# q and k of the first four units by one transfer each, the maximum of k from two turned rows, embeddings later, new order tables

## What is computed

```python
# attention: q, k, v are [8 batches, 8 heads, 576, 64]
q_s = exp(q - max(q, axis=-1)); q_s /= sum(q_s, axis=-1) + 1e-9
k_s = exp(k - max(k, axis=2));  k_s /= sum(k_s, axis=2) + 1e-9
kv = einsum('bhsd,bhse->bhde', k_s, v)
x = einsum('bhsd,bhde->bhse', q_s, kv)      # as rows of 512: 4608 x 512
# first layer: w_in 512 x 2048, w_out 2048 x 512
h = x @ w_in; x = (h - tanh(h)) @ w_out
# routing: cosine with 8 expert embeddings / tau, softmax, the best expert
logits = normed(x) @ normed(emb).T / tau
# second layer: relu(x @ w1[e]) @ w2[e], times the gate, for the rows of expert e
```

## Time and profile before

| | us |
|---|---|
| runs | 1447.04, 1449.97, 1451.49 (median 1449.97) |
| profiled execution | 1449.26 |
| its span, first to last instruction | 1447.2 |
| PE, DVE, ACT, POOL busy | 1413.6, 904.7, 765.1, 396.6 |

### The profile page before, as it was taken

The page is one execution under the profiler, slowest core; times in us unless marked ns, Lnnn a source line. Parts: engine busy times, 40 slices in busy tenths (PEclk is TensorE's granted clock), DMA queues, the critical chain, the costliest instruction groups (busy, mean ns, idle before and its releaser), DMA issues.

```text
span 1447.2 us, 27386 instructions
## 1 busy us (share of the span) xinstructions
PE 1413.6 (98%) x8120; PEld 1218.9 (84%) x8121; DVE 904.7 (63%) x1755; ACT 765.1 (53%) x1574; POOL 396.6 (27%) x346
## 2 busy tenths in 40 slices
PE   6999999999999999999999999999999999999997
PEld 5788888888888888888888888878788888888886
DVE  7986788886688888578888666676314213342111
ACT  5886576666666676657666666663313223242211
POOL 4522253433244443325343323231000000000000
PEclk9999999999999999999999999999999999999999
DMA  9631021221011222002121002035411411411110
GB/s 214 179 93 61 1 72 30 68 50 49 1 47 43 55 50 50 25 1 72 30 68 26 23 1 81 0 103 192 136 44 61 139 44 40 160 36 46 44 38 29
DMA packets 140226, 90.58 MB, mean 63 GB/s; under 512 B 116504, under 2 KB 120856, under 8 KB 139936
## 3 DMA queue, kind: packets, MB, share of 16 engines
q1 hardware_dynamic: 133344, 69.27, 18.5%
q0 software_dynamic: 5840, 18.92, 3.4%
q10 hardware_dynamic: 880, 0.55, 0.1%
HBM read 69.80 MB, written 21.28 MB: 63 GB/s over the span
## 4 chain that ended last, share of the span: by engine, by line
PE 88%; DVE 5%; issue 2%; ACT 2%; DMA 1%; POOL 1%; ACTq 0%; SPq 0%; DVEq 0%; POOLq 0%
PE ps L554 26%; PE ps L555 26%; PE ps L556 25%; PE ps L632 2%; PE ps L752 2%; PE ps L654 1%; PE ps L724 1%; PE ps L643 1%; PE ps L638 1%; DVE gs L1054 1%; PE ps L674 1%; PE ps L625 1%; DMA out<-osb,xrow 1%; PE ps L597 1%; DMA xrow<-scratch 1%
## 5 line engine op out<-in xcount | busy, mean ns | idle before, releaser
L1461 POOL TENSOR_TENSOR g_lo<-gs,g_hi 128x384 fp32r<-128x384 f32 x192 | 199.0, 1037 | 575.4 <-ACT g_hi L851 575.2
L554 PE MATMUL ps<-x_hi,wi_hi 128*128 128x384 f32 x768 | 277.9, 362 | 2.2 <-DVE x_lo L1108 1.1
L555 PE MATMUL ps<-x_lo,wi_hi 128*128 128x384 f32 x768 | 260.0, 339 | 0.0
L556 PE MATMUL ps<-x_hi,wi_lo 128*128 128x384 f32 x768 | 259.9, 338 | 0.0
L841 ACT ACTIVATE usq<-ps 128x384 f32<-128x384 f32 x192 | 94.1, 490 | 290.4 <-PE ps L556 289.8
L554 PE MATMUL ps<-wo_hi,g_hi 128*128 128x512 f32 x576 | 228.4, 397 | 4.4 <-POOL g_lo L1461 3.0
L555 PE MATMUL ps<-wo_lo,g_hi 128*128 128x512 f32 x576 | 229.1, 398 | 0.0
L556 PE MATMUL ps<-wo_hi,g_lo 128*128 128x512 f32 x576 | 227.4, 395 | 0.0
L965 ACT ACTIVATE hb<-ps 128x512 f32<-128x512 f32 x74 | 44.3, 599 | 308.4 <-PE ps L556 303.9
L1051 DVE SCALAR_TENSOR_TENSOR gs<-gs,ps 128x384 f32<-128x384 f32 x192 | 105.8, 551 | 152.0 <-ACT gs L846 151.4
L1054 DVE TENSOR_TENSOR gs<-gs,usq 128x384 f32<-128x384 f32 x192 | 176.7, 920 | 0.0
(11 more groups left out here) (213 smaller groups left out, 2682.0 us busy)
## 6 DMA issues: line engine op xcount, KB each, us to landing
w_raw<-w SPq DMA_DIRECT2D x10, 2048.0 KB, 9.0
xrow<-scratch SPq DMA_DIRECT2D x36, 257.0 KB, 2.7
k_sb<-k SPq DMA_DIRECT2D x60, 144.0 KB, 3.4
q_sb<-q SPq DMA_DIRECT2D x60, 144.0 KB, 3.0
v_sb<-v SPq DMA_DIRECT2D x60, 144.0 KB, 3.4
in_raw<-w_in SPq DMA_DIRECT2D x8, 512.0 KB, 6.8
out_raw<-w_out SPq DMA_DIRECT2D x8, 512.0 KB, 6.0
scratch<-pad_d SPq DMA_DIRECT2D x8, 257.0 KB, 4.4
```

The lines of the kernel that those rows point to most:

```text
L554: mm(out_, a_hi, b_hi, start=first, stop=False)
L555: mm(out_, a_hi, b_lo, start=False, stop=False)
L556: return mm(out_, a_lo, b_hi, start=False, stop=last)
L1461: G.tensor_tensor(g_lo[:, (s - 1) % 3], gs[:, (s - 1) % 2], g_hi[:, (s - 1) % 3].bitcast(F32), ALU.subtract).then_inc(glo_ready, 1)
```

## The change

For units 0 to 3 (`opens`) q and k are loaded by one transfer each, 1536 bytes to a piece, so that in SBUF the 6 rows of one head lie together, and then those of the other: `[96, 2 heads, 6, 64]`. What reads them follows: the maxima and sums over heads, the product with v, and the last step of q on POOL, which writes to a new buffer `q_normal` in the old layout (it lies where `g_hi` is later). Turned, each bank now holds one head of k, two of its rows over the 128 partitions; so `kT` gives a maximum for each bank (128x2), PE turns two rows (128 columns each), and DVE folds the two halves of each into a row `kfold` of 96x128 in SBUF (a reduction over two, 96x256 in PSUM), waits for it, and subtracts that row, read from SBUF, from k. The scratch output of `emb:0` moves from `gs` to a PSUM bank, with a wait for x of the fourth unit. The tables of PE, ACT, DVE and POOL are new; `emb:0`, `emb:1`, `emb:2` are now after `chunk:8`, before `kT:7` and before `chunk:15` on DVE. SP's table is unchanged. ACT's table is left out here: it begins with `qexp:0 qexp:1 row:0 qexp:2 row:1 qa:0 kv:0 qb:0 qa:1 qexp:3 wi:0 out:0` and has no other kinds of work than before.

```diff
         "v:9"),
     PE=order(
-        "kT:0 row:0 kT:1 row:1 kT:2 qa:0 kT:3 qb:0 row:2 qa:1 row:3 kv:0 qb:1 kv:1 kv:2 out:0 qa:2 kv:3 out:1 "
-        "qa:3 qb:2 kT:4 qb:3 out:2 out:3 row:4 chunk:0 chunk:1 qa:4 kv:4 qb:4 chunk:2 out:4 kT:5 chunk:3 "
-        "emb:1 qa:5 row:5 chunk:4 qb:5 kv:5 chunk:5 chunk:6 out:5 chunk:7 kT:6 chunk:8 qa:6 row:6 chunk:9 "
-        "kv:6 qb:6 chunk:10 out:6 chunk:11 kT:7 chunk:12 row:7 chunk:13 qa:7 kv:7 qb:7 chunk:14 out:7 "
-        "chunk:15 chunk:16"),
+        "kT:0 row:0 kT:1 kT:2 kT:3 row:1 kv:0 qa:0 kv:1 qb:0 qa:1 row:2 out:0 row:3 qa:2 qb:1 kv:2 qb:2 qa:3 "
+        "kv:3 out:1 qb:3 kT:4 out:2 out:3 qa:4 row:4 qb:4 chunk:0 kv:4 chunk:1 out:4 chunk:2 kT:5 chunk:3 "
+        "qa:5 row:5 chunk:4 qb:5 kv:5 chunk:5 out:5 chunk:6 kT:6 chunk:7 chunk:8 qa:6 row:6 chunk:9 kv:6 qb:6 "
+        "chunk:10 out:6 chunk:11 kT:7 chunk:12 row:7 qa:7 chunk:13 emb:1 qb:7 kv:7 chunk:14 out:7 chunk:15 "
+        "chunk:16"),
...
     DVE=order(
-        "kT:0 qmax:0 row:0 emb:0 qmax:1 kT:1 qsum:0 row:1 qsum:1 kT:2 qmax:2 kT:3 row:2 qmax:3 row:3 kv:0 "
-        "qsum:2 kv:1 kv:2 qsum:3 out:0 wi:0 kv:3 out:1 qmax:4 kT:4 out:2 out:3 row:4 qsum:4 wi:1 chunk:0 wo:0 "
-        "kv:4 qmax:5 chunk:1 qsum:5 out:4 chunk:2 emb:1 kT:5 wi:2 qmax:6 wo:1 row:5 chunk:3 wo:2 chunk:4 wi:3 "
-        "emb:2 kv:5 qmax:7 wi:4 chunk:5 qsum:6 out:5 chunk:6 wo:3 chunk:7 kT:6 wi:5 row:6 chunk:8 wo:4 wi:6 "
-        "kv:6 chunk:9 qsum:7 wo:5 out:6 chunk:10 chunk:11 kT:7 wo:6 row:7 chunk:12 wi:7 kv:7 chunk:13 "
-        "chunk:14 out:7 chunk:15 wo:7 chunk:16"),
+        "qmax:0 kT:0 qmax:1 row:0 qmax:2 kT:1 qsum:0 row:1 qsum:1 kv:0 qmax:3 kT:2 kT:3 qsum:2 row:2 qsum:3 "
+        "row:3 kv:1 qmax:4 kv:2 out:0 kv:3 wi:0 qsum:4 out:1 kT:4 out:2 out:3 row:4 wi:1 qmax:5 kv:4 chunk:0 "
+        "wo:0 chunk:1 out:4 qsum:5 kT:5 chunk:2 wi:2 wo:1 row:5 chunk:3 wo:2 wi:3 qmax:6 kv:5 chunk:4 chunk:5 "
+        "out:5 qsum:6 chunk:6 kT:6 wi:4 wo:3 chunk:7 qmax:7 wo:4 row:6 chunk:8 emb:0 wi:5 kv:6 chunk:9 qsum:7 "
+        "wo:5 chunk:10 wi:6 out:6 chunk:11 emb:1 kT:7 wi:7 row:7 wo:6 chunk:12 chunk:13 kv:7 out:7 chunk:14 "
+        "emb:2 chunk:15 wo:7 chunk:16"),
     POOL=order(
-        "qmax:0 qmax:1 qsum:0 emb:0 qsum:1 qmax:2 qmax:3 qsum:2 qsum:3 qmax:4 qsum:4 chunk:1 qmax:5 qsum:5 "
-        "chunk:2 chunk:3 qmax:6 chunk:4 chunk:5 qmax:7 chunk:6 qsum:6 chunk:7 chunk:8 chunk:9 chunk:10 "
-        "chunk:11 qsum:7 chunk:12 chunk:13 chunk:14 chunk:15 chunk:16"))
+        "qmax:0 qmax:1 qmax:2 qsum:0 qsum:1 qmax:3 qsum:2 qsum:3 qmax:4 qsum:4 qmax:5 chunk:1 chunk:2 qsum:5 "
+        "chunk:3 chunk:4 qmax:6 chunk:5 chunk:6 qsum:6 chunk:7 qmax:7 chunk:8 chunk:9 emb:0 chunk:10 chunk:11 "
+        "qsum:7 chunk:12 chunk:13 chunk:14 chunk:15 chunk:16"))
...
@@ -252,6 +252,8 @@
 
         return (ps[:, 6:8], ps[:, 0:2], ps[:, 2:4], ps[:, 4:6])[u if u < UPB else 0]
 
+    q_normal = nc.alloc_sbuf_tensor_at("q_normal", [SP, UPB, R, 2 * HD], F32, offset=g_at)
+
     tail_ps = A, Bk, y_ps[1]
     tail_yT = nc.alloc_sbuf_tensor_at("tail_yT", [P, GPB, D], F32, offset=g_at + 9216)
 
@@ -269,6 +271,7 @@
     zeroed, tri_ready = sem("zeroed"), sem("tri_ready")
 
     kfolded, kmaxT_ready, kmax_done = (sem(x) for x in ("kfolded", "kmaxT_ready", "kmax_done"))
+    row_folded = sem("row_folded")
     maxrow_ready, k_centred, k_exp, kv_ready = (sem(x) for x in ("maxrow_ready", "k_centred", "k_exp", "kv_ready"))
     kv_step, kvb_ready = sem("kv_step"), sem("kvb_ready")
     qmax_ready, q_centred, q_exp, q_step, qrec_ready, q_normed = (
@@ -342,15 +345,25 @@
     def arrived(x_in, u, par):
 
         if isinstance(u, int) and u < UPB:
-            return x_in[u], 32
-        return x_in[par], (u - par) * 16
+            return x_in[u], 32 if x_in is v_in else 16
+        return x_in[par], (u - par) * 16 + (0 if x_in is v_in else -16)
 
     def row_count(t, j):
 
         return (t - j) * 4 + 16
 
-    def heads(x):
-
+    def opens(u):
+
+        return isinstance(u, int) and u < UPB
+
+    def per_head(x):
+
+        return x.rearrange("p r c -> p (r c)").rearrange("p (h r d) -> p h r d", h=2, r=R)
+
+    def heads(x, u):
+
+        if opens(u):
+            return per_head(x).rearrange("p h r d -> p (h r) d")
         return x.rearrange("p r (h d) -> p (r h) d", h=2)
 
     def w_piece(w_i, w_o, what, i):
@@ -450,13 +463,15 @@
             freed = i - 1 if i >= 6 else i - UPB + 1
             if what in ("wi", "wo"):
                 load_piece(what, i)
+            elif what in ("q", "k") and opens(i):
+                x_sb, x_d, x_in = (unit_bufs(i, par)[0], q_d, q_in) if what == "q" else (unit_bufs(i, par)[1], k_d, k_in)
+                sp.dma_start(x_sb.rearrange("p r (h d) -> p (r h d)", h=2).rearrange("p (h n) -> p h n", h=2),
+                             x_d[2 * i:2 * i + 2].rearrange("h (p r) d -> p h (r d)", r=R)).then_inc(x_in[i], 16)
             elif what == "q":
-                if i >= UPB:
-                    sp.wait_ge(qTb_ready, freed)
+                sp.wait_ge(qTb_ready, freed)
                 load(unit_bufs(i, par)[0], q_d, q_in, i, par)
             elif what == "k":
-                if i >= UPB:
-                    sp.wait_ge(kv_ready, freed)
+                sp.wait_ge(kv_ready, freed)
                 load(unit_bufs(i, par)[1], k_d, k_in, i, par)
             else:
                 if i == 0:
@@ -588,6 +603,8 @@
         def part(what, u, hf, c, par, t):
 
             q_, k_, v_, kv_, qT_, kfold_, _, _, kmax_, _, bankA, bankB = unit_bufs(u, par)
+            if opens(u):
+                q_ = q_normal[:, u]
             if what == "qa":
                 pe.wait_ge(q_normed, u + 1)
                 pe.wait_ge(kmax_done, u + 1)
@@ -617,8 +634,9 @@
                 pe.wait_ge(kmax_done, u + 1)
                 if not isinstance(u, int) or u >= UPB:
                     pe.wait_ge(xlo_a, earlier(u) if t is None else u)
-                nc.tensor.transpose(bankA[0:SP, 0:P], kmax_[:, 0:1].broadcast_to([P, SP]),
-                                    ident[:]).then_inc(maxrow_ready, 1)
+                for h in range(2 if opens(u) else 1):
+                    last = nc.tensor.transpose(bankA[0:SP, h * P:(h + 1) * P], kmax_[:, h:h + 1].broadcast_to([P, SP]), ident[:])
+                last.then_inc(maxrow_ready, 1)
             elif what == "qb":
                 pe.wait_ge(qTa_copied, u + 1)
                 for r in range(3):
@@ -629,7 +647,8 @@
                 pe.wait_ge(*arrived(v_in, u, par))
                 for r in range(R):
                     for h in range(2):
-                        last = mm(bankA[h * HD:(h + 1) * HD, 0:HW], k_[:, r, h * HD:(h + 1) * HD],
+                        k_rh = per_head(k_)[:, h, r] if opens(u) else k_[:, r, h * HD:(h + 1) * HD]
+                        last = mm(bankA[h * HD:(h + 1) * HD, 0:HW], k_rh,
                                   v_[:, r, h * HW:(h + 1) * HW], start=r == 0, stop=r == R - 1)
                 last.then_inc(kv_ready, 1)
             if what in ("outa", "out"):
@@ -1066,12 +1085,12 @@
                 dve.wait_ge(*arrived(q_in, u, par))
                 if t is None and u >= UPB:
                     dve.wait_ge(q_centred, earlier(u))
-                V.tensor_reduce(qmax_[:], heads(q_), axis=AX.X, op=ALU.max).then_inc(qmax_ready, 1)
+                V.tensor_reduce(qmax_[:], heads(q_, u), axis=AX.X, op=ALU.max).then_inc(qmax_ready, 1)
             elif what == "qsum":
                 dve.wait_ge(q_exp, u + 1)
                 if t is None and u >= UPB:
                     dve.wait_ge(q_normed, earlier(u))
-                V.tensor_reduce(qrec_[:], heads(q_), axis=AX.X, op=ALU.add).then_inc(q_step, 1)
+                V.tensor_reduce(qrec_[:], heads(q_, u), axis=AX.X, op=ALU.add).then_inc(q_step, 1)
                 dve.wait_ge(q_step, u * 2 + 1)
                 V.tensor_scalar_add(qrec_[:], qrec_[:], 1e-9).then_inc(q_step, 1)
                 dve.wait_ge(q_step, u * 2 + 2)
@@ -1081,10 +1100,21 @@
                 V.tensor_reduce(kfold_[:], k_.rearrange("p r c -> p c r"), axis=AX.X, op=ALU.max).then_inc(kfolded, 1)
             elif what == "kT":
                 dve.wait_ge(kmaxT_ready, u + 1)
+                if opens(u):
+
+                    V.tensor_reduce(kmax_[:], both_banks(u)[:, :, 0:HALF], axis=AX.X, op=ALU.max).then_inc(kmax_done, 1)
+                    return
                 turned = bankB[:, 0:SP] if t is not None else both_banks(u)[:, :, 0:HALF]
                 V.tensor_reduce(kmax_[:, 0:1], turned, axis=AX.X if t is not None else AX.XY, op=ALU.max).then_inc(kmax_done, 1)
             elif what == "row":
                 dve.wait_ge(maxrow_ready, u + 1)
+                if opens(u):
+                    V.tensor_reduce(kfold_[:], bankA[0:SP, 0:2 * P].rearrange("p (h i d) -> p h d i", h=2, i=2),
+                                    axis=AX.X, op=ALU.max).then_inc(row_folded, 1)
+                    dve.wait_ge(row_folded, u + 1)
```

(16 more changed lines are left out.)

## The result

The changed kernel takes 1458.87 us (1457.0 to 1461.5), the kernel before, run beside it, 1450.05: the ratio is 1.0062 with a 95% interval of 1.0051 to 1.0074. It is 8.8 us slower. I had forecast 1450.5 and no measurable difference, with 1454.5 as the upper end.

The account below looks back on a forecast made before the run. Bound: DVE's list of work plus its holes up to `chunk:5`, then PE. `out:3` at 36.0 plus 23.15 put `chunk:5` at 59.15; plus 0.4 behind it, 1.2 us later than before, so 1450.5 us, range 1445.5 to 1454.5.

Parts of the forecast that it names:

- DVE's list: DVE's work from `qmax:0` to `out:3`: 23.0 us of known parts plus 1.6 for four folds, 24.6 us.
- the hold-up: Four subtractions with two SBUF inputs wait for POOL's running operation, 1.11 us each, 4.4 us in all.
- rival 1: DVE's subtraction isn't held up because POOL gives way; 3.4 us earlier, 1445.9 us; chance 0.18.
- The 0.2 for `wi:0`: On DVE in the opening, `wi:0` meets POOL's half of `qmax:4` and takes 0.2 us longer.
- The row at 51.07: Earlier profile row, POOL's 3.74 us operation, read as running while DVE's `wo_lo` at 52.73 took its normal 1.20.
- The landing: q:0's arrival before `qmax:0`: longer runs bring it 1.3 us earlier, at 6.8 and not 8.1.
- I count no hole: Up to `out:3`, DVE was taken never to stand idle; the old order had 3.5 us of holes before 32.88.
- My 36.0: End of `out:3` on DVE: 6.8 + 24.6 + 4.4 + 0.2 = 36.0, against 32.88 before.
- 59.15: Forecast start of `chunk:5`'s first product on PE, against 58.32 before.
- 23.15: Time from `out:3` to `chunk:5`, with DVE as the late engine; it was 25.44 us before.
- Behind it: After `chunk:5`: only `emb:1` on PE adds, 0.4 us; the embeddings on DVE are hidden by its holes.
- rival 3: After `chunk:5`, PE begins to wait for weights, `wi:4` onward: 4.4 us more, 1454.9 us; chance 0.15.

Follow-up runs that it names:

- e12: The changed kernel with mixed tables (new up to `chunk:4`, then the old order, embeddings late), folded row still in SBUF: 7.8 us over the kernel before.
- e6: The changed kernel with the folded row in PSUM, new tables up to `chunk:4`, then the old order with embeddings late: 0.2 us over the kernel before.
- e1: The changed kernel with the folded row written to PSUM and read from there by the subtraction: 4.1 us over the kernel before.
- e5: The changed kernel with the old order tables and the folded row in PSUM: 0.5 us over the kernel before.
- e2: The changed kernel with all five old order tables and `emb:0`'s old scratch, folded row in SBUF: 6.3 us over the kernel before.
- e3: The kernel before with the new tables alone (`emb:0`'s scratch in PSUM as they need): 6.6 us over the kernel before.
- e4: The changed kernel with `wi:4`, `wo:4`, `wi:5` and `wo:7` moved earlier in DVE's table only: 8.4 us over the kernel before.
- e8: The changed kernel with only `wo:7` moved ahead of `chunk:15` on DVE: 1455.90 us, 5.6 over the kernel before.
- e7: The changed kernel with the folded row in PSUM and two transfers each for q and k of a unit: 2.9 us over the kernel before.
- e9: The changed kernel with row in PSUM, mixed tables, two transfers each for q and k, `qmax:6` earlier, `wo:7` ahead of `chunk:15`: 0.6 us under the kernel before.

## Why the prediction was wrong

**DVE's list and the hold-up were right.** The fold took 0.36 to 0.41 (forecast 0.40) and the subtraction 2.00 to 2.05 (0.94 + 1.11). e12 against e6 shows that these hold-ups cost 4.75 us, so rival 1 (no hold-up) is out. The 0.2 for `wi:0` did not come: it took 1.21. The Trainium skill's rule in SBUF — State Buffer, "Who interferes with whom", holds in all four cases: POOL's operation began 0.23 to 0.29 us before the subtraction and lasted its 1.47, and the subtraction waited. The row at 51.07 in the earlier trace rows, which spoke for rival 1, I had misread. POOL was not at work when `wo_lo` began at 52.73; it was held itself, since another two-input instruction of DVE was running when it came:

```profile
50.74 1.20 DVE L1190 TENSOR_TENSOR wi_lo<-in_raw,wi_hi 128x1024 fp32r<-128x1024 f32 x1
```

POOL's 3.74 end at 54.81, 0.9 us after `wo_lo`'s end, and 0.9 is about what its g_lo takes by itself. Why it didn't get in between the two, while DVE's `qmax` ran from 51.87 to 52.80, stays open.

**The landing was mis-sized, and so were the holes, and they cancelled.** q:0 was there at 5.33 and not at 6.8. I had priced the landing by the rate alone and left out when the transfers are issued. SP's timeline of the kernel before, and then of the changed one:

```profile
2.17 1.30 SPq L427 DMA_DIRECT2D q_sb<-q  x2
```

```profile
1.16 0.44 SPq L468 DMA_DIRECT2D q_sb<-q  x1
```

q:0 was all issued by 3.47 before and by 1.60 now: 1.9 of the 2.8 us by which `qmax:0` starts earlier. And the rate that I took as nearest, 371, is not what the stretch from 10 to 12 us shows. It has 260 GB/s, with 281 of its 580 packets short ones, so the long ones' own rate is somewhat above that. The line of that view, of the changed kernel:

```profile
DMA packets 580, 0.52 MB, mean 260 GB/s; under 512 B 281, under 2 KB 580, under 8 KB 580
```

And "I count no hole" was wrong: DVE waits 1.47 us for q:1 at 8.41, and 0.42, 0.18 and 0.55 later. 5.33 + 24.6 + 4.4 + 0.2 + 2.6 is 37.1, which is where `out:3` ended (36.65 + 0.46). My 36.0 was 1.1 short: 1.5 too late a start, 2.6 of holes left out. That these two nearly cancelled is luck.

**`chunk:5` came out at 59.01 against 59.15, in part by luck.** From `out:3` it took 21.9 and not 23.15, and this cancelled the 1.1. I had taken DVE for the late engine there; but PE worked 21.70 of the 21.91 us and DVE 20.35, so it was PE's list that set the time.

**The step that failed is "Behind it": +0.4, where 8.2 came.** I argued that PE never waited behind 58.32 and that DVE had 6.6 us of holes there. Holes are no reserve unless they lie before the step in question: from 58.33 to the end of `wi:4` at 75.29 DVE now has none over 0.2 us. This is rival 3's ground, to which I had given 0.15. Its first named place, `wi:4`, is there: PE waits 0.9 for it at 75.35. But I priced four eighths of w_in and `emb:0`, 4.4 us, and left out w_out, POOL's table, and the clock. By the runs the 8.2 us are made up so:

- The new order behind `chunk:5`: 5.3. It is the distance from `chunk:5` to `chunk:18` in e1 (68.85) less that before (63.57), with no fall of the clock in it. PE's waits are 3.7 of it (4.8 less 1.1), `emb:1` on PE 0.4; 1.2 I could not assign. With the old order the distance is 63.58 (e5) and 63.55 (e2).
- The clock's fall at 122.7: 1.5. It is 70.40 in the changed kernel less 68.85 in e1, which has the same four waits and no fall.
- Behind `chunk:18`: 1.4, of which scatter can be about 1.

One reason for the new order's loss is the same hold-up that I had found and then looked for in the opening only. The new table sets weights' parts next to each other on DVE while POOL has work. DVE's timeline of the changed kernel:

```profile
52.24 1.20 DVE L1220 TENSOR_TENSOR wi_lo<-in_raw,wi_hi 128x1024 fp32r<-128x1024 f32 x1
53.36 2.03 DVE L1220 TENSOR_TENSOR wo_lo<-out_raw,wo_hi 128x1024 fp32r<-128x1024 f32 x1
...
58.33 1.20 DVE L1220 TENSOR_TENSOR wo_lo<-out_raw,wo_hi 128x1024 fp32r<-128x1024 f32 x1
59.46 2.04 DVE L1220 TENSOR_TENSOR wi_lo<-in_raw,wi_hi 128x1024 fp32r<-128x1024 f32 x1
...
74.08 1.21 DVE L1220 TENSOR_TENSOR wi_lo<-in_raw,wi_hi 128x1024 fp32r<-128x1024 f32 x1
75.21 2.04 DVE L1220 TENSOR_TENSOR wo_lo<-out_raw,wo_hi 128x1024 fp32r<-128x1024 f32 x1
```

and POOL's at the last of these pairs:

```profile
74.24 1.93 POOL L1491 TENSOR_TENSOR g_lo<-gs,g_hi 128x384 fp32r<-128x384 f32 x1 [1.92 <-ACT g_hi L870]
```

POOL came while the first part ran, waited for its end, and took its turn; the second part then waited for POOL, 0.83 us more three times. In the kernel before none of the 16 parts took over 1.23; it has one such pair, at 80.43 and 81.55, while POOL is at rest. e3, with these tables and nothing else of the change, has the same three parts at 2.03 to 2.04. DVE has no hole over 0.2 us from the second pair on, so its 0.83 arrives at PE's wait for gs at 65.24 (0.7) and, with 0.8 at 69.51 (1.01 for an instruction of 0.17) and 0.6 at 71.57 (1.17 for one of 0.54), both beside POOL, at the wait for wi_lo at 75.35 (0.9). The third pair's delay comes behind that `wi_lo` and has no part in it. This is read from the rows; no run took the pairs apart and left the rest, though in e4, with `kT:6` in the third pair, its second part took 1.36.

It also goes the other way. The wait for g_lo at 83.74 (1.4) has this in front of it on POOL, held by DVE's `wo_lo` that began at 80.18:

```profile
80.34 2.39 POOL L1499 TENSOR_TENSOR q_sb<-q_sb,qmax 96x768 f32<-96x768 f32 x1 [4.17 <-DVE qmax L1088]
```

It takes 0.9 over its usual 1.47. The kernel before has such a one too, at 64.04, but no wait of PE behind it.

The last and longest wait, for wo_lo at 121.44 (1.8, before 1.1), has another reason, a place in the table that I had not looked at. The new table has `out:7` ahead of `chunk:14` on DVE, the old one behind it, and DVE stands at `out:7`:

```profile
114.13 0.46 DVE L1134 TENSOR_TENSOR x_lo<-ps,x_hi 128x288 fp32r<-128x288 f32 x1 [4.38 <-ACT x_hi L899]
```

From there it has `out:7`, `chunk:14`, `emb:2` and `chunk:15` to do before `wo:7`, with no hole over 0.2. `emb:2` is hidden, as I had said, where the old order is kept: in e6 it stands ahead of `chunk:15` too, and the wait is 1.0. This too is read from the rows; no run moved `out:7` alone.

**The clock** fell twice, and I had not reckoned with it. The changed kernel's first fall:

```profile
24.00:26.00 2.00, 1.15 (x30) 0.96 (x27) 1.90 (x6) 1.43 (x3) 0.26 (x1) 1.00 1.02 344
26.00:28.00 2.00, 1.31 (x14) 0.78 (x8) 2.00 (x2) 0.00 (x0) 1.22 (x1) 0.82 1.10 296
28.00:30.00 2.00, 1.05 (x21) 1.04 (x22) 1.93 (x8) 1.90 (x5) 0.76 (x1) 0.50 1.12 318
30.00:34.00 4.00, 4.00 (x24) 3.21 (x22) 3.47 (x9) 3.19 (x9) 1.26 (x2) 0.50 1.20 262
```

PE had waited much of the time before it, while DVE was held up. e4, e8 and e12, which have the SBUF row and these tables up to `chunk:3`, have it near 27 or 28 too; e2, with the old ones, doesn't. This one costs little at most: `chunk:5` moved by 4.75 from e6 to e12 for 4.4 of hold-ups, and the difference of 0.35 includes it. The second fall follows the wait of 1.8, but e1 and e7 have that wait without a fall. What decides between them no run shows.

**Forecast chances.** A slower kernel by over 0.3% had 0.12. The range's upper end, 1454.5, took rival 3 at nearly its 4.4. With rival 3's ground at its real size the sum is 1449.3 + 1.2 + 4.9 (the 5.3 less the 0.4 counted already) + 1.5, which is 1456.9, and the 1.4 behind `chunk:18` come on top.

## What to carry to other kernels

An order written out for several engines is one piece: a step moved forward on one engine takes another's turn on a second one, as in e6 and e9, where the wait that was taken away came back in front of g_lo. e4 adds that a wait which has grown can bring a fall of the clock with it. So where a change brings new tables, walk the whole of them, and count for each step on the busiest engine what must be there by when; the idle time of a stretch as a sum says nothing. And before an operand is moved from PSUM to SBUF, look at what the engine that shares the way to SBUF does at that moment: one edit of the fold's place was worth 3.7 to 5.3 us at `chunk:5` here (e1, e12, e5), more than the new transfers and layout brought with the row in PSUM (1.6 under the new tables, 0.4 under the old ones).

## What the runs showed of the hardware

- The DVE instruction with two SBUF inputs waits for a POOL operation that reads SBUF and began before it, up to 1.1 us of its 1.47; with one input in PSUM the same instruction takes 0.95 beside it. If DVE's instruction began first, POOL's waits: 2.39 and not 1.47 at 80.34. Two such DVE instructions in a row let POOL in between them, and the second took 2.03 to 2.04 and not 1.20.
- Runs of 256 bytes went at 207 GB/s. For those of 1536 bytes the stretches scatter: 260 from 10 to 12 us in the changed kernel, with 281 of 580 packets under 512 bytes, and 325 from 8 to 10 us in e7, with 75 of 498. Eight transfers of 288 KB issued 0.45 to 0.5 us apart took long to land: 8.7 us against 5.1 for the same q when each was split in two and issued over a longer time.
- In the changed kernel the granted clock fell to 0.5 for about 3.6 us after a wait of 1.8, PE having worked 1.26 of the 2.70 us before. This cost 1.5 us more than the wait itself. In e1 and e7 the same wait left it at 1.00.
- Up to 139 us two traces of one kernel agree to 0.02 us at every chunk; behind the loop's first turn they differ by 0.6, behind its second by 1.2.
